# Sums reordered, weight copies split and mixing moved to ScalarE and GpSimd in an mLSTM, MLP and experts kernel

## The reference, cut to what matters

```python
h = x @ w_in
x = (h - np.tanh(h)) @ w_out
p = domain_probs / (domain_probs.sum(-1, keepdims=True) + 1e-09)
out = np.zeros((N, D), dtype=np.float32)
for e in range(E):
    h = np.maximum(x @ w1[e], 0.0)
    out += p[:, e:e + 1] * (h @ w2[e])
```

## Time and profile before

| | us |
|---|---|
| median of 3 runs | 593.54 (593.45 to 594.47) |
| the profiled execution | 593.63 |
| its span, first to last instruction | 591.8 |
| PE busy | 568.5 (96%) |
| DVE, ACT, POOL busy | 339.1, 243.7, 246.9 |

### The profile page before, as it was taken

The page is one execution under the profiler, slowest core; times in us unless marked ns, Lnnn a source line. Parts: engine busy times, 40 slices in busy tenths (PEclk is TensorE's granted clock), DMA queues, the critical chain, the costliest instruction groups (busy, mean ns, idle before and its releaser), DMA issues.

```text
span 591.8 us, 10081 instructions
## 1 busy us (share of the span) xinstructions
PE 568.5 (96%) x3796; PEld 540.6 (91%) x3796; DVE 339.1 (57%) x662; ACT 243.7 (41%) x502; POOL 246.9 (42%) x238
## 2 busy tenths in 40 slices
PE   9999999999999999999999899999899999899997
PEld 8999999999998788989899799899899899899897
DVE  6656556565545765587554654554654554654644
ACT  5775655555335454552145322245322244321221
POOL 4888233332203864690067830067830068810000
PEclk9999999999999999999999999999999999999999
DMA  7977445662252012410012210012220012000101
GB/s 282 344 274 249 133 125 149 165 183 69 51 138 69 1 58 59 105 32 35 1 29 88 59 59 1 2 34 83 59 58 2 2 42 74 1 0 1 68 1 68
DMA packets 46359, 48.08 MB, mean 81 GB/s; under 512 B 21830, under 2 KB 36422, under 8 KB 46310
## 3 DMA queue, kind: packets, MB, share of 16 engines
q1 hardware_dynamic: 46208, 47.39, 26.6%
q10 hardware_dynamic: 102, 0.05, 0.0%
HBM read 41.12 MB, written 4.73 MB: 77 GB/s over the span
## 4 chain that ended last, share of the span: by engine, by line
PE 80%; DVE 12%; ACT 4%; issue 3%; SPq 1%; DMA 0%; DVEq 0%; ACTq 0%
PE bank L1690 7%; PE bank L1691 7%; PE bank L1692 7%; PE bank L1665 6%; PE bank L1668 5%; PE bank L1666 5%; PE bank L1667 5%; PE bank L1647 4%; DVE x L1345 4%; PE bank L1649 3%; PE bank L1648 3%; PE bank L1619 3%; PE bank L1620 3%; PE bank L1618 3%; DVE g_tiles L1339 2%
## 5 line engine op out<-in xcount | busy, mean ns | idle before, releaser
L1027 ACT ACTIVATE g_tiles<-x 128x384 fp32r<-128x384 f32 x96 | 50.4, 525 | 193.2 <-DVE x L1345 187.4
L1690 PE MATMUL bank<-fast_w,g_tiles 128*128 128x320 f32 x384 | 119.1, 310 | 0.0
L1691 PE MATMUL bank<-fast_w,g_tiles 128*128 128x320 f32 x384 | 118.6, 309 | 0.0
L1692 PE MATMUL bank<-fast_w,g_tiles 128*128 128x320 f32 x384 | 118.6, 309 | 0.0
L1345 DVE TENSOR_TENSOR x<-bank,x 128x384 f32<-128x384 f32 x160 | 88.3, 552 | 48.8 <-PE bank L1668 47.8
L1339 DVE SCALAR_TENSOR_TENSOR g_tiles<-x,g_tiles 128x384 fp32r<-128x384 f32 x96 | 66.8, 696 | 56.1 <-ACT g_tiles L1027 56.1
L825 POOL TENSOR_TENSOR fast_w<-fast_raw,fast_w 128x512 fp32r<-128x512 f32 x16 | 21.3, 1332 | 146.8 <-ACT fast_w L969 146.8
L1691 PEld LDWEIGHTS bank<-fast_w,g_tiles 128*128 128x128 f32 x384 | 72.6, 189 | 0.0
L1690 PEld LDWEIGHTS bank<-fast_w,g_tiles 128*128 128x128 f32 x384 | 72.4, 188 | 0.0
L1692 PEld LDWEIGHTS bank<-fast_w,g_tiles 128*128 128x128 f32 x384 | 72.1, 188 | 0.0
L1292 DVE TENSOR_TENSOR bank<-bank,g_tmp 128x384 f32<-128x384 f32 (+2 forms) x64 | 36.1, 565 | 52.9 <-ACT g_tmp L982 52.6
(11 more groups left out here) (220 smaller groups left out, 1317.9 us busy)
## 6 DMA issues: line engine op xcount, KB each, us to landing
w_raw<-in_w SPq DMA_DIRECT2D x8, 704.0 KB, 6.8
zb<-z SPq DMA_DIRECT2D x10, 512.0 KB, 4.9
feat<-in_feat SPq DMA_DIRECT2D x10, 512.0 KB, 4.0
fast_raw<-in_w SPq DMA_DIRECT2D x16, 320.0 KB
tok<-in_tok SPq DMA_DIRECT2D x10, 484.0 KB, 4.8
fast_raw<-in_w SPq DMA_DIRECT2D x16, 256.0 KB
fast_raw<-in_w SPq DMA_DIRECT2D x32, 128.0 KB
spare<-xg SPq DMA_DIRECT2D x8, 256.0 KB, 2.9
```

What stands on the lines that cost most here:

```text
L1690: mm(out, g_tiles[:, k, 0, c], high_w, start=first, stop=False)
L1691: mm(out, g_tiles[:, k, 0, c], low_w, start=False, stop=False)
L1692: mm(out, g_tiles[:, k, 1, c], high_w, start=False, stop=stop).then_inc(third_done, 1)
```

## The change

- **Order of sums.** VectorE adds product 3 before it makes the low tile of C21; ScalarE makes the high tile of C12 at the start of the next unit. In unit 0, product 7 comes before the last `down_rows`, and `product(1, 1)` waits for the first sum only.
- **x blocks.** High and low parts of the x blocks are spread over other steps and units.
- **Weight copies.** ScalarE copies a piece in two gaps: four blocks and the down weights after `first_product`, the other three blocks after C11. The sums of blocks get a second buffer (`w_sums_too`), and GpSimd adds piece q + 1 before it makes the low parts of piece q. Within `low_weights` the down part comes between the two up parts. The first pieces start from a sum that is made ahead of `add_x(0)`.
- **Mixing.** ScalarE weighs the accumulators (`weigh_part`, into `weighed`), GpSimd adds them to `out_acc` (`add_group`); for expert 0 ScalarE writes `out_acc` itself. The thirds wait for `acc_read`, ScalarE's reading. VectorE still mixes the last group (`mix_last`).

```diff
@@ sums_in, fast_at @@
+            return w_sums[q % 2 if q >= PPU else 0]
-            return (1, 6, 7, 5, 2, 4, 3) if u == 0 else (1, 6, 2, 7, 5, 4, 3)
+            return (1, 7, 6, 5, 2, 4, 3) if u == 0 else (1, 6, 2, 7, 5, 4, 3)
-        high_at = {53: (0, 0), 54: (0, 1), 57: (1, 0), 58: (1, 1), 62: (2, 0), 63: (2, 1)}
+        high_at = {53: (0, 0), 54: (0, 1), 56: (1, 0), 57: (1, 1), 59: (2, 0), 60: (2, 1), 63: (3, 0)}
@@ gpsimd: low_weights(q) @@
-                pool.wait_ge(high_down, q + 1)
-                G.tensor_tensor(w[:, F_DN + 2 * D:F_PIECE], raw[:, RAW_DN:RAW_PIECE], w[:, F_DN:F_DN + 2 * D].bitcast(F32),
-                                ALU.subtract).then_inc(fast_down, 1)
+                    if part == 0:
+                        pool.wait_ge(high_down, q + 1)
+                        G.tensor_tensor(w[:, F_DN + 2 * D:F_PIECE], raw[:, RAW_DN:RAW_PIECE],
+                                        w[:, F_DN:F_DN + 2 * D].bitcast(F32), ALU.subtract).then_inc(fast_down, 1)
+            def add_group(v):
+
+                for tt in range(TPH):
+                    out = out_acc[:, place(v % HALVES * TPH + tt), :]
+                    pool.wait_ge(acc_read, TPH * v + tt + 1)
+                    after(pool, mixed, TPH * (v - 2 * HALVES) + tt + 1)
+                    G.tensor_tensor(out, out, weighed[:, tt, :], ALU.add).then_inc(mixed, 1)
...
             for q in range(PPU, FAST):
-                add_weights(q)
+                if q + 1 < FAST:
+                    add_weights(q + 1)
+                if q % PPU == 0 and q > PPU:
+                    add_group(HALVES * (q // PPU - 1))
                 low_weights(q)
+                if q % PPU == 2 and q > 2 * PPU:
+                    add_group(HALVES * (q // PPU) - 1)
+            add_group(HALVES * (EXPERTS - 1))
@@ scalar @@
+            def weigh_part(v, tt):
+
+                e, n = v // HALVES, v % HALVES * TPH + tt
+                act.wait_ge(third_done, 12 * (PPU * v + PPU - 1) + 7 + tt)
+                p = probs[:, place(n), e:e + 1]
+                if e == 0:
+                    A(out_acc[:, place(n), :], e_acc(tt)[:, 0:D], ACT.Copy, scale=p).then_inc(acc_read, 1)
+                else:
+                    after(act, mixed, TPH * (v - 1 - HALVES) + tt + 1)
+                    A(weighed[:, tt, :], e_acc(tt)[:, 0:D], ACT.Copy, scale=p).then_inc(acc_read, 1)
@@ vector, units from 1 on @@
                 add_product(u, 4, sum_c, sum_a)
-                low_tile(u, C21, sum_c)
-                if u > PPU - 1 and u % PPU == 0:
-                    for tt in range(TPB, TPH - 1):
-                        mix(u // PPU - 1, tt)
                 dve.wait_ge(summed, 5 * u + SUM_C21)
                 add_product(u, 3, sum_a, sum_a)
+                low_tile(u, C21, sum_c)
                 low_tile(u, C12, sum_a)
@@ tensor @@
-                    pe.wait_ge(mixed, TPH * (u // PPU - 1) + tt + 1)
+                    pe.wait_ge(acc_read, TPH * (u // PPU - 1) + tt + 1)
...
-                pe.wait_ge(summed, 5 * (u - 1) + SUM_C21)
+                pe.wait_ge(summed, 5 * (u - 1) + (SUM_U2 if u == 1 else SUM_C21))
```

More of the change, by code:

```diff
@@ L223, in mlstm_mlp_experts @@
         fast_raw = over("fast_raw", [P, FAST_RING, RAW_PIECE], F32, home["w_raw"])
-        w_sums = over("w_sums", [P, 2, 3 * P], F32, home["w_raw"] + 4 * FAST_RING * RAW_PIECE)
+        w_sums = (over("w_sums", [P, 2, 3 * P], F32, home["w_raw"] + 4 * FAST_RING * RAW_PIECE),
+                  over("w_sums_too", [P, 2, 3 * P], F32, behind + 4 * 5 * 3 * WIDE))
         x2 = over("x2", [P, 5, TOK], F32, home["x_hi"])
@@ L359, in mlstm_mlp_experts @@
         mixed = sem("mixed")
+        acc_read = sem("acc_read")
+        last_mixed = sem("last_mixed")
         dve_step = sem("dve_step")
@@ L806, in add_weights @@
             def add_weights(q):
-                second, third, fourth = (w_sums[:, :, k * P:(k + 1) * P] for k in range(3))
+                second, third, fourth = (sums_in(q)[:, :, k * P:(k + 1) * P] for k in range(3))
                 pool.wait_ge(fast_in[q % FAST_RING], 64 * (q // FAST_RING + 1))
@@ L1029, in _, with copy_weights @@
+            def copy_weights(u):
+                q = fast_at[u]
+                high_weights(q, 0)
+                high_of_down(q)
             for u in range(E_UNITS):
+                if u:
+                    act.wait_ge(summed, 5 * (u - 1) + SUM_C12)
+                    high_tile(u - 1, C12, half_sums[:, (u - 1) % 2, :])
                 first_product(u)
+                v = u // PPU - 1
+                ends = u >= PPU and u % PPU == 0
+                if u > PPU and u % PPU == 1:
+                    weigh_part(v, TPH - 1)
@@ L1055, in _ @@
-                act.wait_ge(summed, 5 * u + SUM_C12)
-                high_tile(u, C12, half_sums[:, u % 2, :])
+                if ends:
+                    weigh_part(v, 4)
+            act.wait_ge(summed, 5 * (E_UNITS - 1) + SUM_C12)
+            high_tile(E_UNITS - 1, C12, half_sums[:, (E_UNITS - 1) % 2, :])
         @block.vector
@@ L1345, in add_product @@
                 V.tensor_tensor(out, bank_of(u, name)[:, 0:WIDE], other, ALU.add).then_inc(summed, 1)
-            for u in range(E_UNITS):
+            sum_a = half_sums[:, 0, :]
+            dve.wait_ge(first_copied, 1)
+            add_product(0, 6, sum_a, sum_a)
+            dve.wait_ge(summed, SUM_U2)
+            add_product(0, 7, sum_b, sum_a)
+            dve.wait_ge(summed, SUM_U3)
+            add_product(0, 5, sum_b, sum_b)
+            low_tile(0, C11, bank_of(0, 2)[:, 0:WIDE])
+            add_product(0, 4, sum_c, sum_a)
+            dve.wait_ge(summed, SUM_C21)
+            add_product(0, 3, sum_a, sum_a)
+            evac(len(L1_SIZES) - 1)
+            low_tile(0, C22, sum_b)
+            low_tile(0, C21, sum_c)
+            low_tile(0, C12, sum_a)
+            for u in range(1, E_UNITS):
                 sum_a = half_sums[:, u % 2, :]
@@ L1714, in _ @@
             product(0, 1)
+            pe.wait_ge(x2_main, 2 * len(L1_SIZES) - 2)
+            product(0, 7)
             down_rows(L1_STEPS - 1)
```

118 lines of the change are left out of this document (53 added, 65 removed).

## The result

| | before | after |
|---|---|---|
| median, four runs each (us) | 593.69 (593.45 to 594.47) | 586.68 (585.15 to 588.12) |
| profiled execution, its span (us) | 593.63, 591.8 | 588.12, 586.3 |

The ratio of the times is 0.9879, 95% interval 0.9853 to 0.9906: 7 us, or 1.2%, faster, where 19.5 us were forecast. The profiled execution is the longest of its four, 1.4 above the median, and 14.0 above the forecast 574.1. Those 14.0 are what has to be found.

What follows compares the result with a forecast made beforehand. It took PE to be bound by stalls, 25.3 us in 31 units, not its clock. Gains of 17.6 in units, 1.4 and 0.5 make 19.5: 593.6 - 19.5 = 574.1 us, range 571 to 577 (55%).

Steps and rivals of the forecast that it cites:

- What bounds the kernel: On PE: clock full in all 40 slices, so the limit is stalls between instructions, 25.3 us in 31 units.
- Part 1: Mixing leaves VectorE: 7.1 us gained in four unit pairs such as 4 and 5, 5.4 in units 8, 16, 24.
- Part 2: Weight copies in two gaps: gain 9.8 us in pairs such as 6, 7 and 8, 9; units 8 and 9 below 21.
- Part 3: Order of sums and x blocks: units 1 to 3 lose 2.9 us before the change; gain 1.8.
- I leave 1.1: Units 1 to 3: 1.1 us of stall stays, from VectorE's low parts of x blocks while GpSimd runs.
- The 1.0 for contention: All 18 units with GpSimd work: low tiles late beside GpSimd's instructions cost 1.0 us in all.
- Part 4: GpSimd's fourth piece is late: product 1 waits 2.5 us at unit 11, 3.1 at unit 19, together 5.6.
- Part 5: Before the experts: gain 1.4 us from first product to unit 1, net 0.5 before it, bounds 1.7 and -1.
- the first: Rival: GpSimd is not late at units 11 and 19, so those stalls vanish, 568.5 us; 17%.
- the second: Rival: GpSimd's blocking costs 0.35 us in each of 18 units instead of 1.0 in all, 579.4 us; 16%.
- The third: Rival: slow adds between pieces 10 and 11, 14 and 15; gain gone from 2.55 us an add; 3%.
- The last: Rival: ScalarE, 2.8 us busier in units with mixing, delays tiles as VectorE did; 11 us less gain, 585; 6%.

Runs made afterwards that it cites:

- x_quiet: Changed kernel with GpSimd's pieces in pairs, x blocks placed later where GpSimd is quiet, its weight sums after them, one product sum earlier: 569.68 us, ratio 0.9588 to before.

## Why the prediction was wrong, point by point

The 14.0 us between the forecast and the profiled execution:

| where | forecast | measured | difference |
|---|---|---|---|
| first product starts at | 233.7 | 235.72 | +2.0 |
| first product to unit 1 | 6.8 | 6.9 | +0.1 |
| units 1 to 3, less the 2.73 of unit 2 | 31.6 | 35.6 | +4.0 |
| units 4 to 9, 20 to 31 and the rest | floor + 1.0 | floor + 1.2 | +0.2 |
| units 10 and 18, over the floor (waits for GpSimd) | 5.6 | 6.1 | +0.5 |
| half clock, units 2, 11, 19 (2.73 + 1.66 + 2.80) | 0 | 7.2 | +7.2 |

These add up to 14.0. In the last three lines the floor of 10.18 a unit is taken off. Another 0.5 us of the half clock lies in unit 1, which ends 0.95 us into it, and is in the line of units 1 to 3.

- **What bounds the kernel: the step that failed most.** It said that the clock is full in all 40 slices, "so neither the clock nor another engine's total is the limit". True of before, where no wait of the stage was above 1.0. But the same text then forecast new waits of 2.5 and 3.1 and priced each at its own length. So the step that failed is this reading of the clock: it was carried over from a trace without long waits to a forecast with two. The text never asked what a wait of that size does to the clock, and the trace of before could not tell. In after, 1.6 to 2.8 us more came with each: a wait of 2.36 cost 4.0, one of 3.42 cost 6.2. The sum put this at nothing without a reason; it should have been named as a term not known. It is 7.2 of the 14.0 us.
- **Part 1 (mixing)** held: 12.9 for 12.5 measured alone. A weighing took 0.52 for the 0.47 assumed, and units 4 and 5 are at the floor.
- **Part 2 (copies in two gaps)** held: units 8 and 9 take 20.42, below the 21 named as the test; 23.03 with the mixing gone alone.
- **Part 3 (sums and x blocks)** failed by its term "I leave 1.1". The order of the sums is right. The x blocks were costed by VectorE's time beside GpSimd; that B11's low part needs ScalarE's high part, and that one a load issued only in unit 1, was not followed, nor that the change itself puts off that load by 3.3 us. Units 1 to 3 idled 4.5 for the 1.1 left. A step that is moved earlier has to be followed back through all of its inputs, the DMA among them. The 1.0 for contention in the other units is near what they cost: low tiles read from SBUF got slower (779 ns on average against 700 in the earlier trace rows), and units 4 to 31 lie 1.2 over the floor beside the waits and the half clock, 0.54 of it in unit 15. That all of it is contention is not shown.
- **Part 4 (GpSimd late)** held in nearly all: down parts at 6.8, 21.2, 36.4 and 51.2 for 6.9, 21.7, 36.5 and 51.3; the fourth piece at 53.4 for 53.5; units 10 and 18 over the floor by 2.5 and 3.6 for 2.5 and 3.1, and next to nothing ahead of unit 27 (0.17). The 30 adds had a median of 0.88 for the 0.87 assumed, but the six between pieces 10 and 11 took 6.01 for 5.2, which is more than the 0.5 missing at unit 19:

```profile
426.08 6.01 POOL L864 TENSOR_TENSOR arena<-arena,x 128x320 f32<-128x320 f32 x6
```

- **Part 5 (before the experts)** failed by the term of -1 to 1.7: it took a gain of 0.5 and the first product was 1.5 later (234.21 in the earlier trace rows, 235.72 now), beyond the lower bound, as in all five profiled executions with this order. The other term held: from the first product to unit 1 it is 6.94 for 8.23, a gain of 1.3 for 1.4. The predicted wait of ScalarE for GpSimd's sums is there, and two more that it did not name: low parts of x beside GpSimd's low parts take 1.82 for a block's tail, and PE's down rows wait 0.43, 0.86 and 0.60 for VectorE, one example each of the engines:

```profile
210.99 1.06 ACT L996 ACTIVATE fast_w<-fast_raw 128x1024 fp32r<-128x1024 f32 x1 [1.88 <-POOL w_sums L826]
```

```profile
215.26 1.82 DVE L1324 TENSOR_TENSOR xa<-arena,xa 32x384 fp32r<-32x384 f32 x1
```

```profile
214.68 0.50 PE L1696 MATMUL bank<-g_hi,w_all 128*128 128x512 f32 x1 [0.86 <-DVE g_lo L1358]
```

- **The rivals.** GpSimd was late, so the first fell; the second, that each unit with GpSimd work pays for the port, fell too: it asked for 6.3 us in 18 units, and units 6 to 9 are at the floor. The third, the slow add, fell at 1.0 in the six of its place. The last, that ScalarE would delay the tiles, fell with the units at the floor; that its 585 lies near the measured 586.68 is chance. None named what happened: a wait for a DMA in unit 1, and half clock with the long waits.

With GpSimd's queue and the x blocks mended (`x_quiet`), the kernel takes 569.68, 17.0 less than after and 4.4 less than the forecast, which had left room for waits of GpSimd that the other order doesn't have.

## What to carry to other kernels

In a forecast with a new wait of TensorE of some 2 us or more, take its length as the lower bound and 1.6 to 2.8 us more as the upper: here half clock came with nine of eleven such waits. Look for it in units that are busy all the time and still long. When a step is moved earlier in a queue, follow every input back to the DMA that brings it, and ask which semaphore that DMA's issue waits for. When the slots of a ring are asked for in turn with the work that needs them, two pieces in a row can hide a load that one by one would wait for.
